# Two row tiles of expert 0 are computed while the last tokens are routed; the opening of attention in another order

## The reference

```python
# q, k, v: (4, 8, 576, 64); k and v are averaged over 8 neighbouring keys (576 -> 72)
scores = scale * q @ k_p.T ; attn = exp(scores - max) / (sum + 1e-9) ; x = attn @ v_p
x = x.transpose(0, 2, 1, 3).reshape(2304, 512)               # tokens x width

# stage B: top 2 of 8 experts
noisy = x @ w_gate + log1p(exp(x @ w_noise)) * noise
top2 = the two largest of noisy, top2_w = softmax over them
out[t] = sum over its experts e of top2_w * relu(x[t] @ w1[e]) @ w2[e]    # 512 -> 1024 -> 512

# stage D: 4 experts, all tokens
out = sum_e p[:, e] * relu(out @ w1[e]) @ w2[e]
```

## Time and profile before

| | us |
|---|---|
| median of 3 runs | 1411.35 (1409.48 to 1411.98) |
| the profiled execution | 1418.43 |
| its span, first to last instruction | 1416.7 |
| PE busy in the span | 1348.5 (95%) |
| DVE busy | 700.4 (49%) |
| ACT busy | 394.0 (28%) |
| POOL busy | 693.4 (49%) |

### The profile page before, as it was taken

One profiled execution on the slowest core, in us unless ns is written; L12 is line 12 of the kernel. 1 busy time (PEld: TensorE's weight loads), 2 busy tenths in 40 slices (PEclk: granted clock), 3 DMA queues, 4 the chain that ended last, 5 costly groups with the idle time before them and its releaser, 6 DMA issues.

```text
span 1416.7 us, 22026 instructions
## 1 busy us (share of the span) xinstructions
PE 1348.5 (95%) x6985; PEld 1186.7 (84%) x6986; DVE 700.4 (49%) x1292; ACT 394.0 (28%) x736; POOL 693.4 (49%) x464
## 2 busy tenths in 40 slices
PE   5992999999999999999999999999999999999997
PEld 4992788888888888878789889899899899989986
DVE  4786422222121222315876685855555655555564
ACT  2561212122212221413343443422222222222210
POOL 1244398274462928397877676442333222233202
PEclk9995999999999999999999999999999999999999
DMA  9948233252333426212323232210011000000002
GB/s 248 282 166 334 75 128 127 84 163 74 131 99 104 134 70 210 84 60 89 99 75 105 90 104 74 82 53 31 30 45 44 30 30 30 30 30 30 14 0 89
DMA packets 63604, 133.71 MB, mean 94 GB/s; under 512 B 5496, under 2 KB 23048, under 8 KB 63448
## 3 DMA queue, kind: packets, MB, share of 16 engines
q1 hardware_dynamic: 43320, 84.69, 18.5%
q0 software_dynamic: 8272, 26.49, 5.8%
q10 hardware_dynamic: 11952, 21.76, 4.7%
HBM read 108.22 MB, written 30.74 MB: 98 GB/s over the span
## 4 chain that ended last, share of the span: by engine, by line
PE 50%; DVE 2%; issue 1%; ACT 0%; DVEq 0%; ACTq 0%
PE banks L1025 26%; PE banks L998 23%; DVE hD L1809 1%; DVE acc L1852 0%; PE banks L984 0%; DVE block_sums L1826 0%; ACT hD L1337 0%; DVE acc L1855 0%; DVE block_sums L1832 0%; DVE x_ops L1805 0%; ACT acc L1227 0%; DVE block_sums L1823 0%; DVE x_sums L1786 0%; ACT unit_w L1359 0%; DVE block_sums L1820 0%
## 5 line engine op out<-in xcount | busy, mean ns | idle before, releaser
L1025 PE MATMUL banks<-unit_w,hD 128*128 128x512 f32 x1728 | 404.7, 391 | 3.2 <-DVE acc L1852 2.5
L1025 PEld LDWEIGHTS banks<-unit_w,hD 128*128 128x128 f32 x1728 | 322.2, 188 | 73.0 <-DVE acc L1852 7.1
L998 PE MATMUL banks<-x_ops,unit_w_hi 128*128 128x384 f32 x1344 | 342.3, 335 | 5.9 <-issue 2.6
L998 PEld LDWEIGHTS banks<-x_ops,unit_w_hi 128*128 128x128 f32 x1344 | 243.3, 188 | 11.5 <-issue 5.4
L1852 DVE SCALAR_TENSOR_TENSOR acc<-banks,sorted_record,acc 128x512 f32<-128x512 f32 x270 | 200.5, 748 | 104.4 <-PE banks L1025 101.5
L878 PE MATMUL banks<-expert_w,xT 128*128 (+1 forms) x960 | 230.7, 396 | 1.5 <-DVE xT L1588 1.5
L533 POOL TENSOR_TENSOR unit_w_lo<-raw_weights,unit_w_hi 128x512 fp32r<-128x512 f32 (+1 forms) x60 | 63.1, 1072 | 339.4 <-ACT unit_w_hi L1353 339.3
L904 PE MATMUL banks<-expert_w,hT 128*128 (+1 forms) x960 | 226.3, 392 | 2.7 <-issue 2.7
L998 PE MATMUL banks<-x_ops,unit_w_lo 128*128 128x384 f32 x672 | 225.1, 335 | 0.0
L904 PEld LDWEIGHTS banks<-expert_w,hT 128*128 128x128 f32 x960 | 181.2, 189 | 40.6 <-issue 3.0
L878 PEld LDWEIGHTS banks<-expert_w,xT 128*128 128x128 f32 x960 | 178.4, 189 | 38.5 <-issue 2.2
(11 more groups left out here) (232 smaller groups left out, 1278.0 us busy)
## 6 DMA issues: line engine op xcount, KB each, us to landing
raw_weights<-in_w SPq DMA_DIRECT2D x32, 1024.0 KB
raw_weights<-in_w1b SPq DMA_DIRECT2D x32, 512.0 KB
raw_weights<-in_w2b SPq DMA_DIRECT2D x32, 512.0 KB, 3.3
x_rows<-x_sorted ACTq DMA_DIRECT2D x43, 256.0 KB, 2.7
y_sorted<-y_rows ACTq DMA_DIRECT2D x40, 256.0 KB
qT<-in_q SPq DMA_DIRECT2D x3, 1152.0 KB, 23.0
kv_half<-in_k SPq DMA_DIRECT2D x5, 576.0 KB, 12.7
kv_half<-in_v SPq DMA_DIRECT2D x5, 576.0 KB, 12.3
```

What stands on the lines that cost most here:

```text
L998: mm = pe.matmul(dst[:, 0:HALF], (w1h, w1l)[st][par][:, b, c, :], x2o[blk][:, a, mv, c, :], start=(first and t == 0), stop=(t == 5), skip_ ...
L1025: mm = pe.matmul(bank[5 + t % 3][:, :], hD[:, buf, st, c, P * t:P * t + P], w2o[par][:, mv, D * c:D * c + D], start=(n == 0), stop=(n == 3 ...
```

## The change

Four things change.

1. **Early tiles.** `EARLY = 2`: the first 256 rows of expert 0's list get places of their own, and only tokens of the first three groups (tiles 0-11, `EARLY_TOKENS = 12`) may lie in them. If these were fewer than 256 rows, the rest would stay filled by a new copy of 0.5 MB on SP's queue; in this input the first 12 tiles have 417 for expert 0. For that, PE counts after group 2 (`early_count`), DVE makes a new base (`late_base`), and group 3's `ranks` waits for it. As soon as the scatters of tiles 0-11 have landed, SP loads the two row tiles, and they are computed between the last routing steps. The table then starts with tile 2, and POOL skips no wait in `tile_b`. `TILES_B` becomes 45, and the y fill 17 tiles in three copies.
2. **Order of the engines' steps** around them, as the rows below show. The memory of `qT` and `kv_half` moves to the end of the region, so that the early tiles' buffers lie over what attention is done with first.
3. **Opening.** q of batch 0 is loaded whole ahead of k of batch 1, q of batch 1 is split in two loads, and `max_subtract(1)` goes ahead of `kv_pool(0, 1)`.
4. **The rest.** On ACT the last softplus goes ahead of the exponential of group 4, and `high_first(3)` (out of the loop's step 19) and the last two exponentials go behind the first `x_hi`. `SORTED` becomes 17 (from 15): 17 indirect stores of records and results, and one plain result store in place of three.

```diff
-SORTED = N // P - 3
+SORTED = N // P - 1
...
             kv_load(0, 0)
-            q_load(0, end=Q_FIRST, signal=q_first_in)
+            q_load(0, end=Q_FIRST[0], signal=q_first_in[0])
             kv_load(0, 1)
...
+            q_load(0, first=Q_FIRST[0])
             kv_load(1, 0)
-            q_load(0, first=Q_FIRST)
+            q_load(1, end=Q_FIRST[1], signal=q_first_in[1])
             kv_load(1, 1)
-            q_load(1)
+            q_load(1, first=Q_FIRST[1])
...
-            for i, (first, end) in enumerate(((DONE_TILES - 6, DONE_TILES + 2), (DONE_TILES + 2, TILES_B))):
+            for i, (first, end) in enumerate(((DONE_TILES - 6, DONE_TILES + 2), (DONE_TILES + 2, TILES_B - 1), (TILES_B - 1, TILES_B))):
...
+            sp.wait_ge(sc_ps, NT)
+            for i in range(XS):
+                sp.wait_ge(xs_out[i], 32 * len(range(i, EARLY_TOKENS, XS)))
+            for j in range(EARLY):
+                sp.dma_start(xg[:, j, :], x_sorted[P + P * j:2 * P + P * j, :]).then_inc(xg_in[j], 16)
...
+            def late_base():
+
+                dve.wait_ge(early_ps, 1)
+                then(dve.tensor_tensor(bump8[:, 0, :], early8[:, :], count_cols, ALU.subtract))
+                then(dve.tensor_scalar(bump8[:, 0, :], bump8[:, 0, :], 0.0, None, ALU.max))
+                dve.tensor_tensor(base_late[:, :], base8[:, :], bump8[:, 0, :], ALU.add)
...
             kv_pool(0, 0)
             max_subtract(0)
+            max_subtract(1)
             kv_pool(0, 1)
...
-            x_lo(0, 1)
             done_tiles()
             y_places()
-            b_step(0, 0)
+            y_copy(0, 1)
+            x_lo(0, EARLY)
+            x_lo(0, EARLY + 1)
+            b_step(0, EARLY)
```

More of the change, by code:

```diff
@@ L631, in tile_b @@
                         nslot = pool.snap((e + 1) % 2, min_val=0, max_val=1)
-                        if not (isinstance(j, int) and j == 0):
-                            pool.wait_ge(y_ps, first)
+                        pool.wait_ge(y_ps, first)
                         src = raw[:, r % 2, :]
@@ L960, in _ @@
             x_turn(0, 0)
+            for g, (first, end) in enumerate(GROUPS[:-1]):
+                if end + 3 >= NT + 2:
+                    ranks(g)
             up(0, 0)
+            ranks(len(GROUPS) - 1)
+            x_turn(0, 1)
+            h_turn(0, 0)
+            count()
+            up(0, 1)
+            order()
+            down(0, 0)
+            h_turn(0, 1)
+            down(0, 1)
+            x_turn(0, EARLY)
             pe.wait_ge(tab_ok, 1)
-            x_turn(0, 1)
-            for u in range(UNROLL_B):
+            codes[EARLY] = load_code(pe, EARLY)
+            up(0, EARLY)
+            x_turn(0, EARLY + 1)
+            for u in range(EARLY, UNROLL_B):
                 b_step(0, u)
@@ L1169, in _ @@
                     high_first(HIGH_AT[s])
-            for g, (first, end) in enumerate(GROUPS[:-1]):
-                if end + 3 >= NT + 2:
-                    second_exp(g)
             softplus(len(GROUPS) - 1)
-            second_exp(len(GROUPS) - 1)
             codes = {}
@@ L1239, in b_step @@
                 h_hi(g, u)
-                if not (start and u == 0):
-                    y_store(g if u else g - 1, (u - 1) % 4)
+                y_store(g if u else g - 1, (u - 1) % 4)
                 x_hi(g + (u + 2) // 4, (u + 2) % 4)
@@ L1279, in _ @@
             x_hi(0, 0)
-            act.wait_ge(rows_ok, 1)
-            x_load(0, 1)
-            relu(0, 0)
-            x_load(0, 2)
-            x_hi(0, 1)
-            x_load(0, 3)
-            for u in range(UNROLL_B):
-                b_step(0, u, start=True)
-            act.wait_ge(y_filled, 32)
+            high_first(3)
+            for g, (first, end) in enumerate(GROUPS):
+                if end + 3 >= NT + 2:
+                    second_exp(g)
+            relu(0, 0)
+            x_hi(0, 1)
+            h_hi(0, 0)
+            relu(0, 1)
+            h_hi(0, 1)
+            act.wait_ge(first_ok, 1)
+            row = act.value_load(first_row[0:1, 0:1], min_val=0, max_val=EXPERTS * CAP - P)
+            act.wait_ge(fronts_in, 16)
+            for i in range(XS):
+                act.wait_ge(xs_out[i], 32 * len(range(i, NT, XS)))
+            act.dma_start(xg[:, EARLY, :], x_sorted[bass.ds(row, P), :]).then_inc(xg_in[EARLY], 16)
+            act.wait_ge(rows_ok, 1)
+            x_load(0, EARLY + 1)
+            y_store(0, 0)
+            for u in range(EARLY):
+                x_load(1, u)
+            x_hi(0, EARLY)
+            x_hi(0, EARLY + 1)
+            relu(0, EARLY)
+            for u in range(EARLY, UNROLL_B):
+                b_step(0, u)
+            act.wait_ge(y_filled, 48)
             with act.Fori(1, SURE_GROUPS - 1) as g:
@@ L1608, in _ @@
                         pair_weights(g)
+                if s == EARLY_TOKENS + 5:
+                    late_base()
                 for r, half in LOW_AT.get(s, ()):
@@ L1627, in _ @@
             dve.tensor_copy(first_row[:, :], front[0:1, 0:1]).then_inc(first_ok, 1)
+            low_half(3, 1)
+            h_lo(0, 0)
             dve.tensor_tensor(sq8[:, :, :], lower8[:, :, :],
@@ L1659, in _ @@
                               cmax.to_broadcast([P, SORTED, EXPERTS]), ALU.is_equal).then_inc(class_ok, 1)
-            for half in range(2):
-                low_half(3, half)
             then(dve.tensor_reduce(t44[:, 0, :], behind, AX.X, ALU.add))
@@ L1683, in _ @@
             dve.tensor_copy(order_i[:, :], order_f).then_inc(order_ok, 1)
-            x_lo(0, 0)
+            h_lo(0, 1)
+            y_copy(0, 0)
             for r in range(4):
@@ L1696, in _ @@
             then(dve.tensor_copy(t44[:, 8, :], t44i[:, 1, :]))
+            then(dve.scalar_tensor_tensor(out=t44[:, 1, :], in0=behind[:, :, 0], scalar=float(EARLY), in1=t44[:, 1, :],
+                                          op0=ALU.mult, op1=ALU.add))
             then(dve.tensor_scalar(t44[:, 1, :], t44[:, 1, :], 1.0, None, ALU.max))
@@ L1757, in _ @@
             domain_weights()
-            for u in range(1, UNROLL_B):
+            for u in range(EARLY + 1, UNROLL_B):
                 b_step(0, u)
```

182 lines of the change are left out of this document (111 added, 71 removed).

## The result

The changed kernel took 1434.99 us (1434.41 to 1435.34, four runs) against 1411.06 of the kernel before: the ratio is 1.0153, 95% interval 1.0130 to 1.0176. It is slower, as forecast, but by more than three times as much, and outside the range that I gave. Its profiled execution took 1434.7 us, span 1432.8.

What follows compares the result with a forecast made beforehand. PE was taken as the bound, 95% busy, with a 26 us hole between attention and the experts. Delays of 4.2 + 1.6 + 0.6 = 6.4 us on 1411.35 gave 1418 us, range 1406 to 1423.

Steps and rivals of the forecast that it cites:

- T0: Start of the first row tile on PE after attention: 130.8 us against 141.3, bounds 124 to 134.
- The 2 us plus bytes over 436 GB/s: The page's rule for a DMA: a row load would land in 2.6 us, where the forecast took 3.8.
- The zero of the opening's loads: Changed order of the opening's q and k loads: taken as 0, bounds 2 us gained, 1 lost.
- handover: Start of expert 1's first `up`, the sixth: at 208.4 us, 4.2 later than before, bounds 203 to 213.
- the wait ahead of `order`: PE waits for DVE's classes after the second early tile's `up`: 2.7 us.
- clock falls: PE's clock dropping at its waits ahead of `order` and the third `up`: about 1.5 us each, one counted.
- four times 3.6 + 0.2 + 4.6, 33.5, without sorts: POOL's splits of expert 1's weights: from 173.3 to 206.8 us, 1.6 ahead of need.
- B to D: Passage from the experts to stage D: two more skipped steps on ACT and a row load cost 1.6 us.
- End: Last block's fifth tile stored by an indirect DMA instead of a plain one: about 0.6 us.
- D: Rival: expert 1's weights or DVE's chain come late, sixth `up` at 212, total 1422 to 1425 us; chance 0.13.
- B: Rival: the delays cancel, early loads sooner and no clock loss at PE's two waits, total 1412.5 us; chance 0.15.
- C: Rival: early scatters not held by the fill, first row tile at 120, total 1407 or 1405.5 us; chance 0.20.

Runs made afterwards that it cites:

- second profile of before: The kernel before, unchanged, profiled once more; that execution took 1415.5 us.
- fill_late: Changed kernel with the y fill issued on SyncE behind the two early row loads instead of ahead of them; 1422.37 us.
- before_opening: Kernel before with only the changed order of the opening loads and the wait that belongs to it; 1413.54 us.
- gates_early: Changed kernel with VectorE's late gate weights and the norm of the domain weights moved ahead of the second tile's `h_lo`; 1426.27 us.
- pool_halves: Changed kernel with each GpSimd split of 2048 columns written as two of 1024; 1436.78 us.
- pool_tail_cut: Changed kernel with GpSimd's steps for tiles 43 and 44 left out; 1439.23 us.
- tiles43: Changed kernel with 43 steps and table entries instead of 45 on every engine, enough for this input only; 1428.34 us.
- sorted15: Changed kernel with 15 sorted tiles instead of 17, not safe for other inputs; 1434.60 us.
- all_undone: Changed kernel with fill behind early loads, gate weights ahead of `h_lo`, 43 steps and 15 sorted tiles, for this input only; 1401.62 us.
- before_fill_split: Kernel before with its y fill behind expert 1's first two raw pieces and the landing of the fourth row load; 1406.94 us, ratio 0.9958.

## Why the prediction was wrong

The sign was right, the size was not: +6.4 forecast, +23.9 measured. From the second profile of before to the changed one: T0 -7.7, from T0 to the sixth `up` +22.3, from there to the last `down` -0.6 (433.8 to 433.2), to stage D +6.3, at the end +2.9: +23.2.

- **T0 and the opening.** 130.8 forecast, 126.4 measured. The early scatters were through at 121.9, not 127, since the fill began at 100.4 and not at 106.25; the row load took 4.3 us where I took 3.8. So the better T0 is luck of the trace: against the second profile of before T0 won 7.7 us and not 10.5. There the same scatters were through at 120.6, 1.3 us sooner than in the changed kernel, under a fill that began at 98.6. That the fill decides T0 is shown by fill_late. The 2 us plus bytes over 436 GB/s that the forecast held against its 3.8 is stated by that section for DMAs that GpSimd issues; these loads are SyncE's and landed 4.3 and 4.6 us behind their issue. The zero of the opening's loads is shown by before_opening. My 141.3 for the kernel before was 7 us of bad luck, which the text did see in the 7.1 between the profiled execution and the median, and then carried over as "the sum moves both alike". It does not: what is late there is attention, ahead of T0.
- **From T0 to the handover.** Forecast 77.6, measured 85.6, and 76.4 with VectorE's gate weights out of the way. Term by term it held: `up(1)` 12.7 behind T0 (13.2), the wait ahead of `order` 1.4 (2.7), `h_lo` uncovered 2.6 (2.4), `up(2)` 40.3 (42.4). Two clock falls came, at the second `down` (7.32) and the third `up` (7.34, the granted clock is 0.79 from 166 to 174 us), where I counted one. **The step that failed** is the sentence that POOL's splits now run "four times 3.6 + 0.2 + 4.6, 33.5, without sorts": I checked only whether GpSimd would be ready in time (it was, at 200.0), not what its back-to-back splits do to VectorE's small instructions under them. In the kernel before these ran in a gap that GpSimd left by waiting for them. VectorE's gate weights, which stand in no term of the forecast, took 10.2 us for 0.5, TensorE's fourth `down` waited 7.2 and ran slow. That is 9.1 us, shown by gates_early and pool_halves.
- **B to D.** 1.6 forecast for ScalarE's skips, 6.3 measured, another 4.7 us. I read ScalarE's skips from the earlier trace rows and never TensorE's, which has the same steps and made the first sums 3.7 us late; and ScalarE's own term was too small, 3.5 us later measured (from 2.4 to 5.9 behind the last `down`). pool_tail_cut shows that it is not GpSimd, tiles43 that it is the two steps; it does not part TensorE's from ScalarE's.
- **End.** 0.6 forecast from the landing of one store; 2.9 measured. The span does not end with a landing: it ends 10 us behind GpSimd's last indirect store, and two more sorted tiles put that two output tiles of 1.36 us later. sorted15 shows it in this stretch, not in its median.
- **The rivals.** D had the right direction and none of these mechanisms; B and C did not come. With all side costs out and the fill moved the early tiles make a kernel 10 us faster (all_undone), of which moving the fill gives 4.8 without them (before_fill_split); as written, T0 won 7.7 and the routing inside the chain took 13 (76.4 against 63.3).

## What to carry to other kernels

When a change moves work of one engine under a long instruction of another, ask what the two share, and not only whether each is ready in time: here VectorE's small SBUF-to-SBUF instructions belonged where GpSimd waits. Count a loop's added steps on every queue, TensorE's own too, and find what each is hidden under. A run that takes a step from all queues at once says what the step costs, and not on which engine. Before costing anything against a profile that is slower than the median of the runs, find where it lost that time.

## What the runs showed of the hardware

- Instructions of VectorE of 0.16 us took 2.5 to 4.4 us under GpSimd's 128x2048 splits and ended within 0.03 us of them; with 128x1024 splits such small ones took up to 2.24, and six were held instead of three.
- In all kernels the span ended 10.1 to 10.4 us behind the issue of GpSimd's last indirect store, though that store had landed 2.7 us behind its issue. The records show a DRAIN on GpSimd's queue over that time (1422.22 to 1432.56 in the changed kernel); what it waits for they don't show.
- One compare-and-branch on TensorE's queue took 2.18 us (2.53 in pool_tail_cut, 2.05 in fill_late), the others of the changed kernel up to 0.47; in the kernel before none took more than 0.47. In 645 to 657 us three packets moved on the instruction queue. The Trainium skill (Runtime: NRT & Kernel Launch, Instruction fetch mechanics) says that a taken branch out of the fetched pages waits for a transfer; no run here tells that branch apart from others, so this stays a likely reading.
- Attention of the same kernel ended 7.6 us apart in two executions.
